# Expert layers in plain fp32 instead of high and low parts, with W1 blocks stationary and four weight buffers

## The reference

```python
# attention: B, H, S, D = 4, 8, 768, 48
f = 1 / (1 + exp(-f_logit))
for t in range(S):
    state = f[t][:, None] * state + outer(k[t], v[t])
    y[t] = q[t] @ state
x = y as 3072 rows of 384
# first expert layer: E = 8 experts, w1 384 x 1024, w2 1024 x 384
logits = normalised(x) @ normalised(expert_emb).T / tau
e = argmax(logits);  gate = softmax(logits)[e]
x = gate * (relu(x @ w1[e]) @ w2[e])
# second expert layer, own weights
rows with x @ w_skip > 0:  e = argmax(x @ w_gate);  gate = softmax(...)[e]
    out = x + gate * (relu(x @ w1[e]) @ w2[e])
other rows:  out = x
```

## Time and profile before

| | |
|---|---|
| median of 3 runs | 779.96 us (776.52 to 793.05) |
| profiled execution, its own time | 786.7 us |
| its span in the profile | 785.0 us |
| TensorE products | busy 698.8 us, 89% of the span |
| TensorE loads of the stationary operand | busy 628.4 us, 80% |
| DVE | busy 388.7 us, 50% |
| ACT | busy 355.7 us, 45% |
| POOL | busy 388.7 us, 50%, of which the splitting is 234.0 us |
| transfers | 99.42 MB, mean 127 GB/s |

### The profile page before, as it was taken

How to read it: one execution, slowest core, us unless ns; L and a number is a source line. 1 busy time by engine, 2 the same in 40 slices (tenths; PEclk the granted TensorE clock), 3 DMA queues, 4 the chain that set the end, 5 groups by cost and what they waited for, 6 DMA issues and landing times.

```text
span 785.0 us, 16547 instructions
## 1 busy us (share of the span) xinstructions
PE 698.8 (89%) x4912; PEld 628.4 (80%) x4913; DVE 388.7 (50%) x1001; ACT 355.7 (45%) x611; POOL 388.7 (50%) x309
## 2 busy tenths in 40 slices
PE   5889998998719999999999999998399999999992
PEld 4889897997718888788888888887289899898992
DVE  5858988987223554564455555554222222222220
ACT  3556565573205535353534544532254544545420
POOL 4234473543147456563553746641377556658610
PEclk9999999998559999999999999999599999999997
DMA  8675476556530334261423333510454744744110
GB/s 154 158 200 113 83 171 121 129 116 208 188 107 18 126 111 154 86 201 40 134 89 107 129 128 109 179 52 21 152 180 152 228 140 146 229 151 145 51 41 21
DMA packets 147048, 99.42 MB, mean 127 GB/s; under 512 B 109983, under 2 KB 137930, under 8 KB 147008
## 3 DMA queue, kind: packets, MB, share of 16 engines
q1 hardware_dynamic: 140544, 86.19, 38.8%
q0 software_dynamic: 6464, 12.72, 4.5%
HBM read 83.00 MB, written 23.14 MB: 135 GB/s over the span
## 4 chain that ended last, share of the span: by engine, by line
PE 74%; DVE 9%; issue 8%; DMA 3%; ACT 2%; POOL 1%; SPq 1%; ACTq 0%; POOLq 0%; DVEq 0%
PE banks_y L871 9%; PE banks_y L873 8%; PE bank_a L861 8%; PE banks_y L872 8%; PE bank_a L862 8%; PE bank_a L863 8%; PE bank_b L880 5%; PE banks_y L753 4%; PE banks_s L924 2%; PE banks_s L732 2%; PE banks_y L895 2%; PE banks_y L745 2%; DMA raw_f<-in_f_logit 1%; PE banks_y L682 1%; PE banks_s L654 1%
## 5 line engine op out<-in xcount | busy, mean ns | idle before, releaser
L550 POOL TENSOR_TENSOR w_lo<-raw_w,w_hi 128x768 fp32r<-128x768 f32 x128 | 234.0, 1856 | 75.0 <-ACT w_hi L969 68.0
L871 PE MATMUL banks_y<-w_hi,h_hi 128*128 128x384 f32 x384 | 136.4, 355 | 4.7 <-DVE h_lo L1480 4.7
L873 PE MATMUL banks_y<-w_hi,h_lo 128*128 128x384 f32 x384 | 130.5, 340 | 0.0
L872 PE MATMUL banks_y<-w_lo,h_hi 128*128 128x384 f32 x384 | 130.1, 339 | 0.0
L861 PE MATMUL bank_a<-w_hi,x_hi 128*128 128x512 f32 x288 | 127.2, 442 | 3.0 <-DVE x_lo L1474 3.0
L862 PE MATMUL bank_a<-w_lo,x_hi 128*128 128x512 f32 x288 | 115.9, 402 | 0.0
L863 PE MATMUL bank_a<-w_hi,x_lo 128*128 128x512 f32 x288 | 115.8, 402 | 0.0
L1094 ACT ACTIVATE h_hi<-bank_b 128x512 fp32r<-128x512 f32 x96 | 57.4, 598 | 127.7 <-PE bank_b L880 126.5
L1090 ACT ACTIVATE hid<-bank_a 128x512 f32<-128x512 f32 x96 | 57.5, 599 | 106.0 <-PE bank_a L863 104.7
L969 ACT ACTIVATE w_hi<-raw_w 128x768 fp32r<-128x768 f32 x128 | 101.0, 838 | 3.0 <-DMA raw_w<-in_moe_w 3.0
L1480 DVE TENSOR_TENSOR h_lo<-bank_b,h_hi 128x512 fp32r<-128x512 f32 x96 | 66.2, 689 | 61.2 <-ACT h_hi L1094 60.4
(11 more groups left out here) (183 smaller groups left out, 1105.7 us busy)
## 6 DMA issues: line engine op xcount, KB each, us to landing
raw_w<-in_moe_w SPq DMA_DIRECT2D x32, 1536.0 KB, 7.0
xs<-sorted_rows SPq DMA_DIRECT2D x48, 194.0 KB, 5.1
raw_f<-in_f_logit SPq DMA_DIRECT2D x32, 144.0 KB, 2.7
raw_k<-in_k SPq DMA_DIRECT2D x32, 144.0 KB, 2.9
raw_q<-in_q SPq DMA_DIRECT2D x32, 144.0 KB, 3.1
raw_v<-in_v SPq DMA_DIRECT2D x32, 144.0 KB, 2.9
kept<-sorted_rows SPq DMA_DIRECT2D x21, 194.0 KB
sorted_rows<-pad_row SPq DMA_DIRECT2D x16, 194.0 KB, 2.4
```

The lines of the kernel that those rows point to most:

```text
L550: pool.tensor_tensor(w_lo[par][:, sl, :], raw_w[par][:, sl, :], w_hi[par][:, sl, :].bitcast(F32), ALU.subtract).then_inc(w_split_lo, 1)
L871: pe.matmul(ps_out, h_hi[:, kf, :], hi, start=(kf == 0), stop=False)
L872: pe.matmul(ps_out, h_hi[:, kf, :], lo, start=False, stop=False)
L873: ins = pe.matmul(ps_out, h_lo[:, kf, :], hi, start=False, stop=(kf == KF - 1))
```

## The change

The expert layers lose the high and low parts. Weights, rows and hidden rows are plain fp32. In the first product a block of W1 (128 x 128) is stationary and the transposed rows (128 columns) are moving: the result comes out transposed, so the ReLU writes at once what the second product needs as stationary operand, and the eight transposes of the hidden rows go. The memory that is freed makes four weight buffers. Weights come in five pieces an expert (three of W1, 0.5 MB each, two of W2, 0.77 MB each). SP loads three experts' pieces among the pair inputs of the attention stage, from the fifth pair on, and the fourth expert's after it; ACT loads an expert's pieces when the buffer of the one before the current is free. The second product of a tile is run half in its own tile and half after the transposes of the next; the first layer's routing of tile t - 1 lies between the halves of the first product of tile t and after it. On DVE `finish_a` comes before `route_a` and `place_a`, and `place_a` waits for free rows later than before. The loop over experts is written out, and the tiles that are first in a stage no longer run old steps on empty data.

```diff
-        raw_w0 = sb("raw_w0", [P, SLICES, SW])
-        w_hi0 = sb("w_hi0", [P, SLICES, SW], F32R)
-        w_lo0 = sb("w_lo0", [P, SLICES, SW], F32R)
+        w_buf = [sb(f"w_buf{i}", [P, 2 * WELEM]) for i in range(BUFFERS - 1)]
...
+        def load_piece(queue, we, piece):
+            w1, w2 = weights[we // E]
+            buf, e, i = w_buf[we % BUFFERS], we % E, we % BUFFERS
+            if piece < KD:
+                queue.dma_start(buf[:, piece * F:(piece + 1) * F], w1[e, :, piece, :]).then_inc(w1_in[i], 16)
+            else:
+                part = slice((piece - KD) * HKF, (piece - KD + 1) * HKF)
...
+        def first_piece(g):
+            return min(max(0, (g - 4) * 4 // 3), (BUFFERS - 1) * PIECES) if g < PAIRS else (BUFFERS - 1) * PIECES
...
+            for g in range(2, PAIRS):
+                sp.wait_ge(tq_ready, g - 1)
+                load_pair(g, g % 2, v_used=g - 1)
+                for piece in range(first_piece(g), first_piece(g + 1)):
+                    load_piece(sp, piece // PIECES, piece % PIECES)
             sp.wait_ge(y_ready, PAIRS)
-            load_w1(0, 1, 1)
-            load_w2(0, 1, 1)
+            for piece in range(PIECES):
+                load_piece(sp, BUFFERS - 1, piece)
...
-                def expand(par, t, half, kds, s=s):
-                    for kd in kds:
-                        hi, lo = w1_slice(w_hi[par], kd, half), w1_slice(w_lo[par], kd, half)
-                        pe.matmul(ps_h[half], x_hi[:, kd, :], hi, start=(kd == 0), stop=False)
-                        pe.matmul(ps_h[half], x_hi[:, kd, :], lo, start=False, stop=False)
-                        ins = pe.matmul(ps_h[half], x_lo[:, kd, :], hi, start=False, stop=(kd == KD - 1))
+                def expand(we, half, s=s):
+                    for j in range(HKF):
+                        for kd in range(KD):
+                            ins = pe.matmul(ps_h[half][:, j * P:(j + 1) * P], w1_block(we, kd, half * HKF + j), x_cols[:, kd, :],
+                                            start=(kd == 0), stop=(kd == KD - 1), skip_group_check=True)
+                    ins.then_inc(s[f"h{half}"], 1)
+                def contract(we, half):
+                    for kf in range(half * HKF, (half + 1) * HKF):
+                        ins = pe.matmul(ps_out, h_t[:, kf, :], w2_rows(we, kf), start=(kf == 0), stop=(kf == KF - 1),
+                                        skip_group_check=True)
                     return ins
...
+                def tile(e, i, t, first, m=m, s=s):
+                    we, old = e + m * E, has_old(e, first)
                     pe.wait_ge(s["xs_in"], 16 * (t + 1))
                     for kd in range(KD):
                         ins = pe.transpose(ps_xt[:, kd * P:(kd + 1) * P], xs[:, kd * P:(kd + 1) * P], ident[:])
                     ins.then_inc(s["xt"], 1)
+                    if old:
+                        contract_end(we - 1 if first else we, t - 1)
                     if first:
+                        wait_w1(pe, we)
+                    pe.wait_ge(s["x_copied"], t + 1)
+                    expand(we, 0)
+                    if old and m == 0:
+                        route_t(t - 1)
+                    expand(we, 1)
+                    if old and m == 0:
+                        route_logit(t - 1)
+                    if first:
+                        wait_w2(pe, we)
+                    if old:
+                        pe.wait_ge(s["row"], t + 1)
+                    pe.wait_ge(s["relu0"], t + 1)
+                    contract(we, 0)
+                    if old and m == 0:
+                        rank(g, t, 1, ps_rank_1, ps_count_1)
...
+                def load_weights(we, u, s=s):
+                    act.wait_ge(s["y"], u + 1)
+                    settle(act)
+                    for piece in range(PIECES):
+                        load_piece(act, we, piece)
...
+                def tile(e, i, t, first, m=m, s=s):
+                    we, old = e + m * E, has_old(e, first)
+                    act.wait_ge(s["xt"], t + 1)
+                    act.activation(x_cols[:].rearrange("p k x -> p (k x)"), ps_xt, ACT.Copy).then_inc(s["x_copied"], 1)
                     relu(0, t)
+                    if old and m == 0:
+                        route_copy(t - 1)
                     relu(1, t)
+                    if old and m == 0:
+                        softmax_1(t - 1)
+                    if first and old and we - 1 + BUFFERS < 2 * E:
+                        load_weights(we - 1 + BUFFERS, t - 1)
...
                     if m == 0:
+                        finish_a(ch, u)
                         route_a(ch, u)
-                        hidden_low(1, u)
                         place_a(ch, u)
-                        finish_a(ch, u)
```

More of the change, by code:

```diff
@@ L60, in gla_moe_program @@
     KF = F // P
+    HKF = KF // 2
     HALF = F // 2
@@ L347, in x_part_before, with has_old @@
             return x_part(g - 1) if g > 0 else None
-        def first_slice(g):
-            b, hp = g // HP, g % HP
-            return g - 2 if b == 0 and hp >= 2 else 2 * b + hp if b > 0 and hp < 2 else None
-        def unless_first_tile(engine, par, e, first, body):
-            if first and par == 0:
-                settle(engine)
-                with engine.If(e > 0):
-                    body()
-            else:
-                body()
+        def first_piece(g):
+            return min(max(0, (g - 4) * 4 // 3), (BUFFERS - 1) * PIECES) if g < PAIRS else (BUFFERS - 1) * PIECES
+        def has_old(e, first):
+            return e > 0 or not first
         @block.sync
@@ L876, in hidden_t @@
-                def hidden_t(half, t, s=s, freed=None):
-                    pe.wait_ge(s[f"relu{half}"], t + 1)
-                    for j in range(KF // 2):
-                        ins = pe.transpose(ps_ht[half][:, j * P:(j + 1) * P],
-                                           hid[:, half * HALF + j * P:half * HALF + (j + 1) * P], ident[:])
-                        if freed is not None and j == 0:
-                            ins.then_inc(freed, 1)
-                    ins.then_inc(s[f"ht{half}"], 1)
```

346 lines of the change are left out of this document (81 added, 265 removed).

## The result

| | before | after |
|---|---|---|
| median of 4 runs | 782.07 us (776.52 to 793.05) | 818.18 us (815.86 to 828.58) |
| ratio, 95% interval | | 1.0477 [1.0383, 1.0571], slower |
| profiled execution, its span | 786.7, 785.0 | 819.9, 818.2 |
| TensorE products, busy | 698.8 | 750.6 |
| DVE busy | 388.7 | 265.3 |

The kernel became slower by 33.2 us of span. Three engines lost much work, and the one that sets the time gained some. In the page of the changed kernel the chain and the groups of the two products answer to the earlier trace rows and to the removed lines 861 to 873.

What follows compares the result with a forecast made beforehand. TensorE's own work per tile was taken as the bound (74% of the span). Attention -4, first expert stage +18.5 and second +30.3 gave +45 us: 832 for the profiled execution, median 825, range 802 to 872.

Steps and rivals of the forecast that it cites:

- upper corner: Whole kernel: 884 us, with the pass prices of both products and attention at their upper bounds.
- within 2%: Whole kernel: up to 795.6 us, needing the lowest price of both products and the best attention; chance 0.06.
- Passes: Expert products on TensorE: one load with its product takes 0.112 us at 128 moving columns, 0.328 at 384.
- Tile: Expert stages: tile period 12.12 us in the first against 10.68, 11.06 in the second against 9.62; 1.44 more each.
- hand-overs: Each expert tile on TensorE: 0.10 us added between groups of products.
- Switches: Change of expert, seven a stage: the extra 2.0 us falls to an allowance of 0.4, 3 us a stage.
- First tiles: Start of each expert stage: 9.5 us plus half-clock cost of 3.5 or 5.8, so 13.0 and 15.3.
- Drain of the first stage: End of first expert stage: last half product with its wait 2.7 us, then 14.6 to the next stage as today.
- Attention: Attention stage: small weight pieces save 5 us, three pairs may give back 1; net -4, bounds -10 and +5.
- A: Rival, expert products: fp32 is cheaper, one cycle a column per record, tile 8.4 us, about 695 in all; chance 0.06.
- C: Rival, first product: stationary load does not hide under 128 columns, 0.213 us a pass, about 1055 in all; chance 0.04.
- B: Rival, expert switches: ACT, held by its weight issues, copies x some 4 us late at 11 switches, 870; chance 0.12.

Runs made afterwards that it cites:

- late burst: Changed kernel with the 3 MB weight load that ACT issues at the first expert stage's end moved into the second stage's first tile: 818.3 us, ratio 1.0304.

## Why the prediction was right, and where it was not

The forecast was 825 us and +45 of span; measured were 818.2 and +33.2, inside the range, slower as forecast. The mechanism was the one predicted: fp32 passes on a full TensorE. Two slips of the arithmetic touched nothing else: the upper corner is 825 + 54 + 9 = 888 and not 884, and the lowest corner, 799, already lies above the 795.6 up to which 0.06 was given for "within 2%".

- **Passes.** 0.112 and 0.328 us were predicted, 0.1117 and 0.3225 measured. The neighbours in the attention stage gave both: the transpose for 128 columns almost to the digit, and two cycles a column and a little for 384, at 0.320 plus 0.8% where 2.5% was taken. The reason given for the 0.112, that it streams as many columns, was only half of it: with 64 columns it is 0.1106, so it is the load that binds. A product of two such passes of 384 columns takes 0.645 us, 4.03 cycles a column; the four passes of the Trainium skill's page FP8 and Floating Point Precision, section TensorE Precision Notes, would be this number.
- **Tile.** 12.12 and 11.06 were predicted, 11.94 and 10.85 measured. Each is 0.2 too long: 0.09 from the second product, 0.02 from the first, and the rest the hand-overs, which cost nothing. Over 26 and 20 periods that is 4.7 and 4.2 us.
- **Switches.** An allowance of 0.4 us each was left; they cost 0. That is 3 us in each stage. The step before it was right, and the run with DVE splitting shows why: with POOL's subtractions out of the way, TensorE's wait for the small DVE instruction is gone (10.7 us before, 1.4 with it). The 2.0 us a switch were read from one of the cheaper ones; two took 3.7, and the seven together cost 17.6 us over the plain period and not 14.
- **First tiles.** 13.0 and 15.3 were predicted, 10.93 and 585.96 - 573.91 = 12.05 measured, 2.1 and 3.2 us less. The 9.5 us were right: 1.57 to the first product, 5.36 and 2.58. Too large was what half the clock adds, 3.5 and 5.8 predicted, 1.4 and 2.6 measured. One part of the step that failed is that it charged half the clock from the first transposes on, though the 1.5 us up to the first product hold it already (1.57 measured with the clock at half); that is 0.8 us too much in each. The other is that it took the stretch at half clock from the kernel before, until 6.9 us and some 11.6 us after the start of the stage. Windows of the two starts, and behind them the first tile of the repeat of the same kernel:

```profile
235.00:240.00 5.00, 5.00 (x42) 5.00 (x42) 0.00 (x0) 0.60 (x1) 0.00 (x0) 0.91 0.00 0
...
580.00:586.00 6.00, 6.00 (x38) 4.89 (x38) 0.00 (x0) 1.19 (x2) 0.00 (x0) 0.95 0.00 0
```
```profile
232.65 0.90 PE L786 MATMUL banks_s<-ident,xs 128*128 128x128 f32 x3 [14.73 <-DMA xs<-sorted_rows]
...
244.97 0.49 PE L786 MATMUL banks_s<-ident,xs 128*128 128x128 f32 x3
```
```profile
235.00:240.00 5.00, 5.00 (x25) 5.00 (x25) 0.00 (x0) 0.28 (x1) 0.00 (x0) 0.51 0.13 38
```

  A mean of 0.91 over 5 us is 0.9 us at half, so until 235.9, 4.4 us after the start; in the second stage 0.95 over 6 us is 0.6 us, until 580.6, 6.7 after it. But this is not the kernel's own: in the repeat the clock was at half until 7.3 us after the start of the first stage, longer than in the kernel before, and its first tiles took 12.32 and 11.19 us; with the late burst they took 11.53 and 10.96. So part of the 2.1 and 3.2 us is the luck of one execution. The end of the second stage came as forecast, 15.3.
- **Drain of the first stage.** 17.3 predicted, 21.1 measured. The step that failed is "from its end to the next stage as today". The weight issues that ACT makes at the last tile were not followed into the transfers behind them. The experiment with a late burst took 3.9 of the gap away.
- **Attention.** -4 predicted, +0.8 measured. The stall of the earlier trace rows was priced rightly (4.5 us at the fourth pair, 4.4 with small pieces in the kernel before). The step that failed is the sum behind it, "may give back 1 in all": the lead did not last, and a fall of the granted clock, which the sum has at nothing, is where it went. The two pairs of 15.1 and 16.0 us run at half of it. Weight pieces are not needed for that (the kernel before with small pieces lost its lead at 59 GB/s) and not enough (the same attention program kept it at 266 GB/s). What makes the clock fall in one execution and not in the next stays open.

The rivals: A would have needed 384 columns in under 0.23 us, they take 0.3225. C would have needed 0.213 a pass, it is 0.1117. B was closest, and this is how near it came, on ACT's queue and ACT at a switch:

```profile
348.24 0.36 ACTq L260 DMA_DIRECT2D w_buf<-in_moe_w  x1
...
348.63 0.94 ACTq L260 DMA_DIRECT2D w_buf<-in_moe_w  x2
...
349.60 1.38 ACTq L263 DMA_DIRECT2D w_buf<-in_moe_w  x2
...
349.86 0.53 PE L786 MATMUL banks_s<-ident,xs 128*128 128x128 f32 x3
350.22 2.10 PE L760 MATMUL banks_y<-w_buf,h_t 128*128 128x384 f32 x6
...
351.39 0.49 ACT L973 ACTIVATE x_cols<-banks_s 128x384 f32<-128x384 f32 x1 [2.87 <-PE banks_s L786]
```

The five issues took 0.36 + 0.94 + 1.38 = 2.7 us, as in its free case. The copy of x came 1.5 us after the start of the transposes instead of 0.6 and ended at 351.9, while TensorE was in its old half product until 352.8. The cover that B doubted was there, with 0.9 us to spare.

The errors of the expert stages add up: -2.1 - 4.7 - 3 + 3.8 = -6.0 in the first and -3.2 - 4.2 - 3 = -10.4 in the second, and attention's +4.8 the other way: together 11.6 of the 45, which leaves 33. That the sum came out this near is in part luck: the expert stages alone were 16.4 us too long, and attention's miss went the other way.

## What to carry to other kernels

On an engine that is full, price a new form of an instruction by its nearest neighbour elsewhere in the same trace, starts against starts, and ask for each form apart whether the stationary load or the moving columns bind it: here plain fp32 was nearly free with 128 moving columns (and saved the transposes) and dear with 384, so the best kernel uses it for one product and not for the other. Relieving engines that are half idle was worth only what they had held up on the full one, here some 12 us in the first stage, most of it by a single instruction beside GpSimd's subtractions. Follow each moved weight load to the small transfers that go out after it, and do not count a lead gained early in a long stage as gained for the whole until a trace shows it at the stage's end.

## What was not expected of the hardware

- A pass with 64 moving fp32 columns takes as long as one with 128 (0.1106 and 0.1117 us), and so does one with 8 (0.112), as long as the stationary block has 128 columns.
- An 8-element DVE instruction beside GpSimd's subtractions took 2.95 us instead of 0.29, across the end of one subtraction to the end of the next.
- A burst of 3 MB on ACT's queue held back a small transfer on SP's: 6.1 us from the pad rows to the next load instead of 2.2.
- The granted clock fell to half in the middle of a busy attention stage in some executions and not in others of the same program, and rose 4.4 us after the start of the expert stage in one and 7.3 us in another; the same attention program began the expert stage anywhere between 227.4 and 234.9 us. For a kernel of 800 us that is 1%, as much as some of the edits studied here.
